# Loading k, r and the decays already turned by channel, and the gate weights transposed, in a one-core chunked-scan kernel

## What is computed

```python
for t in range(S):                      # S = 768, state is D x D per head, D = 48
    kt, vt, rt, wt = (k[:, :, t], v[:, :, t], r[:, :, t], w[:, :, t])
    cur = np.einsum('bhd,bhe->bhde', u[None] * kt, vt)
    y[:, :, t] = np.einsum('bhd,bhde->bhe', rt, state + cur)
    state = wt[:, :, :, None] * state + np.einsum('bhd,bhe->bhde', kt, vt)
...
h = gelu(x @ w_in)                      # 384 -> 1024, u and v are its halves
v_s = np.einsum('ts,bsd->btd', w_sg, layernorm(v) * g_ln) + b_sg[None, :, None]
x = x + (u * v_s) @ w_out
...
u = x + (relu(x^T @ w_tok1) @ w_tok2)^T
out = u + relu(u @ w_ch1) @ w_ch2
```

## Time and profile before

| | us |
|---|---|
| median of 3 runs | 402.94 |
| lowest and highest | 401.98, 403.27 |
| the profiled execution, device time | 400.82 |
| its span, first to last instruction | 399.3 |

### The profile page before, as it was taken

How to read it: one execution, slowest core, us unless ns; L and a number is a source line. 1 busy time by engine, 2 the same in 40 slices (tenths; PEclk the granted TensorE clock), 3 DMA queues, 4 the chain that set the end, 5 groups by cost and what they waited for, 6 DMA issues and landing times.

```text
span 399.3 us, 6566 instructions
## 1 busy us (share of the span) xinstructions
PE 389.4 (98%) x2520; PEld 363.2 (91%) x2520; DVE 183.7 (46%) x380; ACT 113.1 (28%) x215; POOL 166.8 (42%) x185
## 2 busy tenths in 40 slices
PE   6899999999999999999999999999999999999997
PEld 5799988989899999899999999889998899988996
DVE  5798988667744452405444735334013310133101
ACT  4277644655411020763002221222002210022100
POOL 6687897576225671784999960000000000000000
DMA  9999599543100202002122410000110001100001
GB/s 146 179 219 227 87 198 198 125 94 100 56 25 2 79 14 67 2 0 80 39 78 81 126 35 0 2 0 2 39 39 2 1 2 39 41 0 0 8 33 39
DMA packets 60144, 25.01 MB, mean 63 GB/s; under 512 B 51152, under 2 KB 58192, under 8 KB 60112
## 3 DMA queue, kind: packets, MB, share of 16 engines
q1 hardware_dynamic: 60112, 24.58, 29.2%
HBM read 22.22 MB, written 2.36 MB: 62 GB/s over the span
## 4 chain that ended last, share of the span: by engine, by line
PE 93%; DVE 3%; issue 1%; DMA 1%; POOL 1%; SPq 0%; ACT 0%; DVEq 0%; POOLq 0%
PE bank L1129 25%; PE bank L1130 25%; PE bank L1131 25%; PE bank L1233 4%; PE bank L1188 3%; PE bank L1143 3%; PE bank L1229 2%; PE bank L1270 2%; PE bank L1212 1%; DMA rc<-in_r 1%; PE bank L1198 1%; DVE suf L900 1%; PE bank L1288 1%; PE bank L1330 1%; DVE am L941 0%
## 5 line engine op out<-in xcount | busy, mean ns | idle before, releaser
L803 ACT ACTIVATE ha_hi<-bank 128x512 fp32r<-128x512 f32 x36 | 21.5, 598 | 107.7 <-PE bank L1131 107.7
L1047 DVE SCALAR_TENSOR_TENSOR ha_lo<-bank,ha_hi 128x512 fp32r<-128x512 f32 x36 | 24.9, 692 | 51.0 <-ACT ha_hi L803 51.0
L1129 PE MATMUL bank<-c_hi,ha_lo 128*128 128x384 f32 x144 | 48.2, 335 | 0.0
L1131 PE MATMUL bank<-c_hi,ha_hi 128*128 128x384 f32 x144 | 48.1, 334 | 0.0
L1130 PE MATMUL bank<-c_lo,ha_hi 128*128 128x384 f32 x144 | 48.1, 334 | 0.0
L1131 PE MATMUL bank<-u2T_hi,c_hi 128*128 128x512 f32 x108 | 42.1, 390 | 0.0
L1130 PE MATMUL bank<-u2T_lo,c_hi 128*128 128x512 f32 x108 | 42.1, 390 | 0.0
L1129 PE MATMUL bank<-u2T_hi,c_lo 128*128 128x512 f32 x108 | 42.0, 389 | 0.0
L1052 DVE TENSOR_TENSOR x<-bank,x 128x384 f32<-128x384 f32 x12 | 6.7, 558 | 65.1 <-PE bank L1131 65.1
L1129 PE MATMUL bank<-sg_hi,z_lo 128*128 128x384 f32 x96 | 32.5, 338 | 0.0
L1130 PE MATMUL bank<-sg_lo,z_hi 128*128 128x384 f32 x96 | 32.1, 334 | 0.0
(11 more groups left out here) (145 smaller groups left out, 888.8 us busy)
## 6 DMA issues: line engine op xcount, KB each, us to landing
raw<-in_moe_w_ch SPq DMA_DIRECT2D x12, 384.0 KB, 3.1
kc<-in_k SPq DMA_DIRECT2D x12, 192.0 KB, 4.6
rc<-in_r SPq DMA_DIRECT2D x12, 192.0 KB, 5.2
vn<-in_v SPq DMA_DIRECT2D x12, 192.0 KB, 5.3
raw<-in_moe_w_sg SPq DMA_DIRECT2D x6, 384.0 KB, 4.3
out<-x SPq DMA_DIRECT2D x12, 192.0 KB, 1.9
raw<-in_moe_w_in SPq DMA_DIRECT2D x4, 384.0 KB, 4.9
raw<-in_moe_w_tok SPq DMA_DIRECT2D x4, 384.0 KB, 3.2
```

Of the source, the lines that this page charges most:

```text
L803: sc.activation(ha[0][:, i, :], bank[:, :], ACT.Relu).then_inc(act_out, 1)
L1047: ve.scalar_tensor_tensor(ha[1][:, i, :], bank[:, :], 0.0, ha[0][:, i, :].bitcast(F32), ALU.max, ALU.subtract).then_inc(dve_out, 1)
L1129: te.matmul(dst, left[1], right[0], start=first, stop=False)
L1131: return te.matmul(dst, left[0], right[0], start=False, stop=last)
```

## The change

The launch passes four further tensors, laid out on the host: the decays by channel (`w_turned`, 112 x 512 per chunk), k and r by channel side by side (`kr_turned`, 112 x 1024 per chunk), k and r by step side by side (`kr_rows`, 128 x 768) and v by step (`v_rows`, 128 x 384). `w_sg` is passed transposed. With them:

- `turn_w`, `turn_k`, `turn_r` and the twelve `wsg` jobs leave PE; `take_r`, `take_kt` and the `wsg` casts leave ACT; the `wsg` low parts leave DVE. `w_sg` pieces are handled as other weights: ACT rounds them and POOL subtracts.
- Per chunk, SP issues `w_turned` (229 KB), `kr_turned` (459 KB), `kr_rows` (393 KB) and `v_rows` (197 KB), 1.28 MB, in place of four loads of 197 KB, 0.79 MB. Their rows are 1.5 to 4 KB long instead of 192 bytes. The loads stand in another order, and wait on the scaling steps instead of the transposes.
- The scans read the decays from SBUF and a constant `steps` from PSUM. DVE's `scale_k` and the first `scale_r` read k or r from SBUF instead of PSUM; their other input was and is in SBUF.
- For n = 1 to 4 the old state is added by one more matmul into the bank (`carried`) instead of by a DVE addition. The outputs of n = 0 to 4 alternate between banks 5 and 6. `rku` has two buffers.
- In the first two chunks POOL does `scale_k` and `scale_r` of the next chunk before `diagonal_v`; DVE does `diagonal` of chunks 0 and 1 behind `forward`. The range check is summed without DVE's marking step, before `state(4)`.
- `xT 0 2` stands ahead of `v 0 0` in slot 1 of chunk 5. The last output tile is added and stored in two halves.

```diff
-BY_ACT = ("w_in", "w_out")
+BY_ACT = ("w_in", "w_sg", "w_out")
...
             def load_w(n):
                 if n >= NC + WR:
-                    sp.wait_ge(wt_done, n - WR + 1)
-                sp.dma_start(w_tile(n)[:, :, 0:D], rows(w, n)).then_inc(wz_in[n] if n < NC else w_in_[n % WR], 16)
...
+                    sp.wait_ge(pre_done, NP * (n - WR + 1))
+                sp.dma_start(w_tile(n)[0:QP], w_turned[n]).then_inc(wz_in[n] if n < NC else w_in_[n % WR], 16)
+
+            def load_krT(n):
                 if n >= KR:
...
+                    sp.wait_ge(kp_done, n - KR + 1)
+                    sp.wait_ge(rp_done, n - KR + 1)
+                sp.dma_start(krT[0:QP, n % KR], kr_turned[n]).then_inc(krT_in[n % KR], 16)
+
+            def load_kr(n):
...
+                sp.dma_start(kr[:, n % KR], kr_rows[n]).then_inc(kr_in[n % KR], 16)
...
-            low = {5: [("w_in", 0)], 6: [("w_in", 1)]}
+            low = {5: [("w_in", 0)], 6: [("w_in", 1), ("w_sg", 0)], 7: [("w_sg", 1)], 8: [("w_sg", 2), ("w_sg", 3)],
+                   9: [("w_sg", 4)], 10: [("w_sg", 5)]}
...
-            for n in range(YR):
+            for n in range(2):
+                scale_k(n + 1)
+                scale_r(n + 1)
+                diagonal_v(n)
+                rk_products(n + 1)
+                rku_products(n + 1)
+            for n in range(2, YR):
                 diagonal_v(n)
                 rk_products(n + 1)
                 scale_k(n + 1)
                 scale_r(n + 1)
                 rku_products(n + 1)
...
-                    src = decay_bank(n)[0:QP, PART * p:PART * p + PART][:, ::-1]
-                    ve.tensor_tensor_scan(suf[0:QP, n % 2, p, 0:PART][:, ::-1], src, ones[0:QP, :], 1.0, ALU.mult,
-                                          ALU.bypass).then_inc(suf_done, 1)
+                    ve.tensor_tensor_scan(suf[0:QP, n % 2, p, 0:PART][:, ::-1], w_tile(n)[0:QP, p, :][:, ::-1],
+                                          steps[0:QP, :], 1.0, ALU.mult, ALU.bypass).then_inc(suf_done, 1)
...
-                dve.wait_ge(kt_done, n + 1)
+                wait_ring(dve, krT_in, n)
                 dve.wait_ge(qk_done, n)
                 dve.wait_ge(kn_turned, states(n - 1))
-                ve.tensor_tensor(kp[0:QP, :, :], pairs(b1)[0:QP, :, :], suf[0:QP, n % 2, :, 1:PART + 1], ALU.mult
+                ve.tensor_tensor(kp[0:QP, :, :], krT[0:QP, n % KR, 0], suf[0:QP, n % 2, :, 1:PART + 1], ALU.mult
                                  ).then_inc(kp_done, 1)
...
+                carried = 0 < n < YR
+                if carried:
+                    te.matmul(b1[0:QP, 0:NP * D], ident[0:QP, 0:QP], st[0:QP, :, :].rearrange("c p d -> c (p d)"),
+                              start=True, stop=False)
...
-                elif kind == "wsg":
-                    tt, sh = i // 2, i % 2
-                    wait_raw(pe, ("w_sg", tt))
-                    for j in range(3):
-                        ins = te.transpose(bank[:, tile(j)], raw[:, PIECE_AT["w_sg", tt] % SLOTS, tile(3 * sh + j)],
-                                           ident[:, :])
                 elif kind == "sg":
                     dt, th = i // 2, i % 2
-                    wait_dve_out(pe, "wsg", 0, 11)
+                    wait_split(pe, "w_sg", 5)
```

More of the change, by code:

```diff
@@ L223, in sem @@
             return ctx.enter_context(nc.semaphore(name))
-        w_in_, k_in, r_in, v_in = ([sem(f"{n}_in{i}") for i in range(ring)]
-                                   for n, ring in (("w", WR), ("k", KR), ("r", KR), ("v", VR)))
+        w_in_, kr_in, krT_in, v_in = ([sem(f"{n}_in{i}") for i in range(ring)]
+                                      for n, ring in (("w", WR), ("kr", KR), ("krT", KR), ("v", VR)))
         wz_in = [sem(f"wz_in{i}") for i in range(NC)]
@@ L270, in wait_split @@
         def wait_split(eng, *piece):
-            eng.wait_ge(w_split, SPLIT_AT[piece] + 1)
+            eng.wait_ge(w_split, PIECE_AT[piece] + 1)
         def wait_raw(eng, piece):
@@ L306, in split_target @@
                 return win[part][:, :, 256 * i:256 * i + 256]
+            if name == "w_sg":
+                return sg[part][:, i, :]
             if name == "w_out":
@@ L425, in _ @@
             load_raw(1)
-            later = {3: [2], 4: [3], 5: [4], 6: [5], 7: [6], 8: [7, 8], 9: [9, 10], 10: [11, 12], 11: [13, 14]}
-            for n in range(3, NCH):
-                if n > 3:
-                    if n + 2 < NCH:
-                        load_k(n + 2)
-                        load_r(n + 2)
-                    if n + 1 < NCH:
-                        load_v(n + 1)
-                    if n + 3 < NCH:
-                        load_w(n + 3)
+            later = {4: [2], 5: [3, 4], 6: [5], 7: [6, 7], 8: [8], 9: [9, 10], 10: [11], 11: [12, 13, 14]}
+            for n in range(4, NCH):
+                if n + 2 < NCH:
+                    load_krT(n + 2)
+                    load_kr(n + 2)
+                if n + 1 < NCH:
+                    load_v(n + 1)
+                if n + 3 < NCH:
+                    load_w(n + 3)
                 for i in later.get(n, []):
@@ L933, in diagonal @@
                     dve.wait_ge(base_done, n)
-                ve.tensor_reduce(dg[:, :], rku[:, :, :], AX.X, ALU.add).then_inc(dg_done, 1)
+                ve.tensor_reduce(dg[:, :], rku[:, n % 2].rearrange("p (h d) -> p h d", h=H), AX.X, ALU.add).then_inc(dg_done, 1)
             def mask(n, i):
@@ L1211, in state_products @@
                         q = slice(HP * i, HP if i == 0 else QP)
-                        ins = te.matmul(state_bank(n)[q, D * p:D * p + D], kn[:, p, q], vn[:, n % VR, D * (2 * p + i):D * (2 * p + i + 1)],
-                                        start=True, stop=True)
+                        ins = te.matmul(b1[q, D * p:D * p + D], kn[:, p, q], vn[:, n % VR, D * (2 * p + i):D * (2 * p + i + 1)],
+                                        start=not carried, stop=p == NP - 1 or not carried)
                 ins.then_inc(ds_done, 1)
@@ L1232, in outputs @@
                         h = 2 * p + i
-                        ins = te.matmul(by[:, tile(h, D)], am[:, h, :], vn[:, n % VR, tile(h, D)], start=not inner,
+                        ins = te.matmul(yb[:, tile(h, D)], am[:, h, :], vn[:, n % VR, tile(h, D)], start=not inner,
                                         stop=i == 1 or not inner)
@@ L1237, in sum_range @@
             def sum_range():
-                pe.wait_ge(ok_marked, 1)
-                te.matmul(bc, ones[:, :], okf[:, :], start=True, stop=True).then_inc(ok_summed, 1)
+                pe.wait_ge(checked, CHECKS)
+                te.matmul(bc, ones[:, :], acc[:, :], start=True, stop=True).then_inc(ok_summed, 1)
             def free_bank(job):
```

341 lines of the change are left out of this document (134 added, 207 removed), and 12 rows, old and new, of the table SLOT.

## The result

| | before | after |
|---|---|---|
| median, us | 402.51 (401.98 to 403.27, 4 runs) | 416.94 (416.61 to 417.2, 4 runs) |
| span of the profiled execution, us | 399.3 | 415.1 |
| granted TensorE clock, mean of the span | 1.00 | 0.918 |
| F, start of the flag copy | 45.20 | 62.24 |
| first gate product | 112.22 | 126.74 |

A forecast was written before the change was run, and what follows sets the result against it. TensorE was taken as the bound (93% of the chain), then POOL's queue from the flag copy to the gate product. Gains 5.0 + 5.8 = 10.8 us took 400.82 to 390.0; plus 2.1 gave 392.1 us, range 386 to 397.5.

The forecast's parts named there:

- part 2: Chunks 1 to 4 up to the flag copy, three transpose groups fewer per chunk: 27.05 us instead of 27.4.
- a time that no transpose now fills: Each of chunks 1 to 4: 2.3 us from start of scores to end of ACT's `kn` copy, without transposes.
- S11: Start of the scores of chunk 11, forecast at flag copy + 68.5 us instead of + 74.3.
- S1: Start of the scores of chunk 1, forecast at 13.15 us instead of 17.81.
- Or if the first chunk is held by a load: Failure condition in chunk 0: the forecast fails if a load holds the first chunk; no size given.
- Its longer chunk: One chunk before the flag copy forecast at 7.2 us, because the masks of chunk 2 come about 1.1 us late.
- 0.4 us per contention: Chunks 6 to 11: a full POOL pays 0.4 us beside each of six DVE `scale_k`, 2.4 us in all.
- I cost them at nothing: Loads up to the flag copy: 9.9 MB at 347 GB/s take 28.5 us of 40, so no cost.
- the forecast's last rival: Loads late at 181 GB/s: flag copy near 57.5 us, time 409.4 us, slower than before; chance 0.04.
- The port costs both engines: DVE and POOL delays at `scale_k` add, six times 1.1 us; no gain in chunks 1 to 4: 396.6 us; chance 0.20.
- PE stays the bound: First gate product starts when PE gets there, not held by POOL: 16.9 us gained, 386.0 us; chance 0.12.
- The 2.1 us added at the end: Whole-kernel term: the median of three runs lay 2.1 us above the profiled execution, taking 390.0 to 392.1.

The follow-up runs named there:

- e1_fill: Changed kernel with identity products added in chunk 0: 4 more ahead of the first scores, 12 in the wait for v's first rows; 407.63 us.
- e9_fill_rest: e5_fill_kn with POOL's small `rstd` steps moved off, a `w_in` low part ahead of the flag copy, other waits to chunk 5 and before gate product filled; 392.77 us.
- e8_refill_low: Changed kernel, chunk 0 unfilled, with 8 identity products in each wait for `kn` in chunks 1 to 4; 402.03 us.
- e12_best: e9_fill_rest with the `w_in` low part behind the flag copy again, v's first rows two places earlier, 6 products in chunk 0 instead of 12; 391.09 us.
- e11_fill_more: e6_fill_all with 8 identity products instead of 3 in each wait for `kn`; 397.19 us.
- e15_split_first: e12_best with the last `w_sg` low part ahead of POOL's other steps in chunk 10, and 4 products before the gate product instead of 14; 387.96 us.
- e13_refill_3: e8_refill_low with 3 identity products instead of 8 in each wait for `kn`; 398.64 us.
- e2_v_early: Changed kernel with v's first rows loaded two places earlier, ahead of u and chunk 1's k and r by channel; 414.34 us.
- e5_fill_kn: e1_fill with 3 identity products in each wait for `kn` in chunks 1 to 4; 399.2 us.
- e6_fill_all: e5_fill_kn with 14 identity products ahead of the first gate product, in its own bank; 396.91 us.
- e3_before_gap: Kernel before the change with v's first rows loaded three places later, behind the third chunk's w, k and r; 407.24 us.
- e4_fill_dve: e1_fill with the low parts of the last three `w_sg` pieces made by DVE instead of POOL; 414.89 us.

## Why the prediction was wrong

**The step that failed** is in part 2: "a time that no transpose now fills". I saw that the wait for `kn` was left open, and costed it as its own length. Its length was right (0.67 us, and a chunk of 6.25 us at the high clock for the 6.1 forecast). What failed is that nothing else was costed: neither the sum nor a rival had a term for PE's clock, though the earlier trace rows list it. With that time open the clock stayed at 0.50 to 74.9 us; with three products in it per chunk, twelve in all, it came back at 24.0, and the kernel is 18.3 us faster. Whether the wait or the work that left with the transposes weighs more stays open.

**Where the 26.6 us are.** The forecast's span was 388.5, the measured 415.1. F is 22.0 late, and from F to S11 it took 73.0 in place of 68.5.

- *S1*: 17.04, forecast 13.15. With chunk 0 filled it is 14.84 (e1_fill) and 15.00 (e9_fill_rest), with v earlier too 14.03. So of 3.9 us some 2.0 are clock, 1.0 the late v, 0.9 my sum, of which 0.3 is a slip: the terms as written add to 13.45, not 13.15. "Or if the first chunk is held by a load" was written as what would break the forecast; it happened. The clock fell 0.3 us into that gap; in e8_refill_low it fell at 8.8 us, before the gap, behind 1.80 us ahead of the first scores, so the late v is not shown to be what dropped it.
- *Chunks 1 to 4 and to F*: 45.2 us, forecast 27.05. At the high clock, in e12_best, 27.56: chunks of 6.26, 7.22, 6.27 and 6.45 and 1.36 to F. The sum of part 2 was right to 0.5 us. Its longer chunk is chunk 2, as costed (7.22 for 7.2); 0.7 us of it is filled wait for `am`. 17.6 of the 18.1 us are clock.
- *F to the gate product*: forecast F + 61.2. After: F + 64.5, with the clock low up to F + 13. Where the clock held, F + 60.7 (e11_fill_more). POOL's queue with 0.4 us per contention was sized well: in that run six of its steps are 0.32 to 0.56 us longer than elsewhere, 2.75 us in all, for 2.4. The wait of PE was 3.3, not 6 us: PE itself gets there later than I had it. In e12_best the products of identity in front of the gate product start at 97.73, F + 56.1, where I had F + 55.1; in e11_fill_more, where chunk 5 has no filled waits, at 102.50, F + 57.4.
- *F to S11*: forecast 68.5; 68.0 in e11_fill_more, 73.0 after. All of the miss is clock.
- *The end* is unchanged (279.8 and 279.8), as costed.

**Loads.** "I cost them at nothing" at 347 GB/s was wrong in the rate. 235 to 290 GB/s came over the first chunks (248 in 16:28 after; 290 in 8:41.5 of e12_best). It is not the forecast's last rival either: at the low clock no chunk behind chunk 0 waited for them. At the high one POOL waited up to 3.22 us and PE up to 3.45 us for rows of chunk 3, differently each time, and in e12_best not at all. Why the rate varies stays open.

**Rivals.** "The port costs both engines" stays small in the changed kernel (DVE's `scale_k` took 1.33 and 1.10 in places, 0.66 alone), and "PE stays the bound" is refuted by the idle 3.26 us ahead of the gate product and by e15_split_first. The change's own gain is real where the clock holds (393.0 us of span in e11_fill_more, with products of identity alone); the ratio of 0.966 is that of the change with fills, relief, an earlier load of v and one reordering together, and the relief is worth nothing without the change.

**The 2.1 us added at the end** stand for the distance of the profiled execution from the median, and they are clock as well: beside the runs here the kernel before took 400.65 and 400.68 us at a mean clock of 1.000, 401.8 to 403.4 at 0.996, and 402.8 to 405.0 at 0.991 and 0.992.

## What to carry to other kernels

Work that is taken off TensorE may have been what filled its waits: before removing it, list each wait it covers, and price an uncovered one by the clock too, not by its length alone. If TensorE slows by half, look at the granted clock per stretch before the busy shares, which stay high (96% here). A few products without use in a short wait are cheap insurance, and then the next queue (here GpSimd's) can be shortened in the order of its steps.

## What the hardware showed that I had not expected

**The clock.** With a wait of 0.67 us in each chunk of 10.87 us it stood at 0.50 with PE busy 43.3 of 46.0 us (16:62 after), and stayed there with PE busy 16.68 of 16.75 us behind the last of these waits; with three products in each it was back at 24 us (e13_refill_3). Falls came behind waits of 0.67 and 0.60 us (e1_fill), 1.31 and 0.71 (e2_v_early), 1.80 (e8_refill_low) and 1.21 (e5_fill_kn), and inside waits of 2.58 us (after 0.3 us of it), 3.45 (e6_fill_all, after 0.5), 2.23 (e3_before_gap, near its end) and 3.26 (the gate product, after 2.7). But waits of 0.50 and 0.87 us at 47 to 50 us passed in e6_fill_all, and almost the same at 45 to 47 us (0.51 and 0.87) were followed by 0.50 in e5_fill_kn, so the length of a wait does not settle it alone. The Trainium skill, TensorE: Matmul & The Clock Gate, "A second HAM failure mode: psum-queue depth-cycling", tells of a kernel that cycles through PSUM banks and whose short idle times between groups of matmuls make the clock go to and fro; the traces agree in kind, but here it stayed low. The Trainium skill, TensorE: Matmul & The Clock Gate, "Part 1: The HAM clock gate", puts the penalty of the ramp at under 1% of a typical kernel's span. What was met here is more than a ramp, a clock that did not come back for 65 us, and cost 18.3 of 416.9 us, 4.4%.

**The shared port.** In e4_fill_dve a DVE operation with both inputs in SBUF started while a POOL step ran (92.90 to 94.18) and was held through the next three POOL steps as well, one of 1.84 and two in 2.52: 5.33 us in place of 0.95. The Trainium skill, SBUF — State Buffer, "Who interferes with whom", lets whoever issues first have the shared ports for one whole instruction. By that DVE would have waited for the step that ran, and been ahead of the one that began at 94.14, 0.19 us behind DVE's own start. The row says otherwise, and decides: beside a POOL that goes from step to step DVE's turn did not come.
